# A two-part schedule of a recurrence and dense layers: new order tables, a ring of decay rates with 10 places in place of 11, half as many products of r and v

## The reference

```python
def _attn_ref(r, k, v, w, a, b):            # 4 batches, 8 heads, 768 steps, 40 wide
    state = zeros((B, H, D, D))
    for t in range(S):
        y[:, :, t] = einsum('bhd,bhde->bhe', rt, state)
        Sa = einsum('bhde,bhe->bhd', state, at)
        state_decay = state * wt[:, :, None, :] - einsum('bhd,bhe->bhde', Sa, bt)
        state = state_decay + einsum('bhd,bhe->bhde', vt, kt)
def _moe_ref(x, w_in, w_out):               # 3072 x 320 -> 2048 -> 320
    h = x @ w_in
    g = where(h >= 1, h, where(h <= -1, 0, (h + 1) ** 2 / 4))
    return g @ w_out
def _moe2_ref(x, w1, w2, w3, w_out):        # 3072 x 320 -> 768 -> 320
    return maximum(maximum(x @ w1, x @ w2), x @ w3) @ w_out
```

## Time and profile before

| | us |
|---|---|
| median of 3 runs | 1052.78 |
| lowest, highest | 1052.1, 1056.64 |
| the profiled execution | 1052.78 |
| its span, first to last instruction | 1051.1 |
| TensorE busy | 962.9 (92%) |
| VectorE, ScalarE, GpSimd busy | 506.8, 393.1, 456.5 |
| mean granted TensorE clock | 0.97 of 2.4 GHz |

### The profile page before, as it was taken

How to read it: one execution, slowest core, us unless ns; L and a number is a source line. 1 busy time by engine, 2 the same in 40 slices (tenths; PEclk the granted TensorE clock), 3 DMA queues, 4 the chain that set the end, 5 groups by cost and what they waited for, 6 DMA issues and landing times.

```text
span 1051.1 us, 29793 instructions
## 1 busy us (share of the span) xinstructions
PE 962.9 (92%) x12330; PEld 807.1 (77%) x12330; DVE 506.8 (48%) x700; ACT 393.1 (37%) x719; POOL 456.5 (43%) x633
## 2 busy tenths in 40 slices
PE   6648999899998887899999999999999999999998
PEld 5436787788776776677888788878887888888887
DVE  8886666667552452696333323332333243324321
ACT  1214455455554563464233323332333133313321
POOL 3586786959688841242133213321332133123311
PEclk9957999999998899999999999999999999999999
DMA  5854667676645631462000100010001000100000
GB/s 84 142 108 89 119 104 133 102 139 107 128 81 116 116 72 28 135 181 68 1 26 1 31 1 26 0 30 0 25 0 30 0 25 0 30 0 26 0 1 26
DMA packets 242915, 61.27 MB, mean 58 GB/s; under 512 B 223728, under 2 KB 238832, under 8 KB 242800
## 3 DMA queue, kind: packets, MB, share of 16 engines
q1 hardware_dynamic: 147760, 44.86, 19.3%
q10 hardware_dynamic: 95040, 14.76, 8.6%
HBM read 44.89 MB, written 14.68 MB: 57 GB/s over the span
## 4 chain that ended last, share of the span: by engine, by line
issue 27%; PE 17%; POOL 10%; DVE 3%; ACT 1%; DMA 1%; POOLq 0%; DVEq 0%; ACTq 0%; SPq 0%
POOL hid_lo L1399 10%; PE ring L1212 8%; PE acc L1212 5%; PE ring L1222 3%; PE ring L1254 2%; DVE sq L1457 1%; PE acc L1276 1%; DVE clip L1451 1%; DMA raw<-in_moe_w_dram 1%; DVE wmax_lo L1425 1%; ACT sq L1361 0%; ACT hid_hi L1337 0%; POOLq L35 0%; DVE win_lo L1425 0%; DVE wout_lo L1417 0%
## 5 line engine op out<-in xcount | busy, mean ns | idle before, releaser
L1399 POOL TENSOR_TENSOR hid_lo<-sq,hid_hi 128x512 fp32r<-128x512 f32 x132 | 174.4, 1321 | 453.5 <-ACT hid_hi L1337 453.5
L1451 DVE TENSOR_SCALAR clip<-ring 128x512 f32<-128x512 f32 x96 | 66.2, 690 | 132.1 <-PE ring L1222 132.1
L448 POOL TENSOR_TENSOR prod<-sysX 128x30 f32<-128x30 f32 (+14 forms) x193 | 101.8, 527 | 58.1 <-DMA sysX<-systems 42.8
L1337 ACT CAST hid_hi<-sq 128x512 fp32r<-128x512 f32 x132 | 82.0, 622 | 93.5 <-DVE sq L1457 71.5
L1361 ACT ACTIVATE sq<-clip 128x512 f32<-128x512 f32 x96 | 60.7, 633 | 147.7 <-DVE clip L1451 145.9
L452 POOL TENSOR_TENSOR sysX<-sysX,prod 128x30 f32<-128x30 f32 (+14 forms) x193 | 106.9, 554 | 15.1
L1457 DVE SCALAR_TENSOR_TENSOR sq<-clip,sq 128x512 f32<-128x512 f32 x96 | 67.9, 708 | 59.9 <-ACT sq L1361 59.9
L1212 PE MATMUL acc<-hid_hi,wout_hi 128*128 128x512 f32 x192 | 76.4, 398 | 7.7 <-POOL hid_lo L1399 7.6
L1482 DVE TENSOR_TENSOR sq<-ring,clip 128x512 f32<-128x512 f32 x36 | 24.9, 692 | 120.4 <-PE ring L1222 98.1
L1383 ACT COPY clip<-ring 128x512 f32<-128x512 f32 x36 | 21.1, 587 | 153.8 <-PE ring L1222 153.8
L1212 PE MATMUL ring<-x_hi,win_hi 128*128 128x512 f32 x192 | 75.5, 393 | 3.4 <-PEq L958 3.4
(11 more groups left out here) (166 smaller groups left out, 2177.4 us busy)
## 6 DMA issues: line engine op xcount, KB each, us to landing
nat_k<-in_k_dram ACTq DMA_DIRECT2D x48, 80.0 KB, 3.4
vz<-in_v_dram SPq DMA_DIRECT2D x96, 40.0 KB
nat_r<-in_r_dram SPq DMA_DIRECT2D x96, 40.0 KB, 2.8
xT<-yT SPq DMA_DIRECT2D x96, 40.0 KB
out_dram<-res SPq DMA_DIRECT2D x24, 160.0 KB, 1.8
inverses_T<-sysX SPq DMA_DIRECT2D x7, 512.0 KB, 4.5
nat_w<-in_w_dram ACTq DMA_DIRECT2D x44, 80.0 KB
nat_a<-in_a_dram ACTq DMA_DIRECT2D x44, 80.0 KB, 3.5
```

The lines of the kernel that those rows point to most:

```text
L448: g_.tensor_tensor(some, X[:, 0:j, j:j + 1].to_broadcast([P, j, rest]), X[:, j:j + 1, j + 1:BLK].to_broadcast([P, j, rest]), ALU.mult)\
L1337: nc.scalar.copy(hid[(u if u < T1 else u - T1) % HB][0][:, :], src).then_inc(hid_hi, 1)
L1399: nc.gpsimd.tensor_tensor(hid[at % HB][1][:, :], sq[at % 2][:, :], f32(hid[at % HB][0][:, :]), ALU.subtract)\
L1451: nc.vector.tensor_scalar(clip[f % 2][:, :], ring[(f + 2) % 4][:, :], -1.0, None, ALU.max).then_inc(clipped, 1)
```

## The change: what it does

- ORDER, FINISH, START, SOLVE_FROM, SOLVE_AT, FIRST_STEP and BANK get other contents. Stages w, a, b, n run 9, 8, 8, 8 pieces ahead in place of 10, 9, 9, 9; dn stays at 9 on TensorE and goes from 9 to 8 on VectorE. On GpSimd a round has 12 steps in place of 9, and a unit's solving starts later.
- The ring `rates` has EARLY (10) places in place of 11; every wait that named RATED names EARLY.
- rr does one product with a weight tile of 64 rows and 128 columns where it did two with 64 by 64: 32 products a piece in place of 64.
- VectorE's steps of unit 1 write to a tile of their own, `prod_v`, in place of `xsum`, and the wait of x(0) for these steps is gone. They start one short round earlier.

```diff
-EARLY, RATED, LATE = 10, 11, 3
+EARLY, LATE = 10, 3
-        rates = ring("rates", RATED, [P, RATES + DM])
+        rates = ring("rates", EARLY, [P, RATES + DM])
-        prod = sb("prod", [P, (BLK // 2) ** 2])
+        prod, prod_v = (sb(n, [P, (BLK // 2) ** 2]) for n in ("prod", "prod_v"))
         ORDER = {
-            "PE": [("g", 0), ("p", 0), ("gs", 0), ("qt", 0), ("dn", 9), ("z", 0), ("ys", 0), ("w", 10), ("yt", 0),
-                   ("vz", 0), ("k", 1), ("a", 9), ("r", 2), ("rr", 0), ("b", 9), ("ak", 1), ("st", -1), ("n", 9),
-                   ("xy", 0)],
-            "ACT": [("load w1", 10), ("load b0", 10), ("load b1", 9), ("load k0", 2), ("rates", 0), ("load k1", 2),
-                    ("p", 0), ("gs", 0), ("qt", 0), ("inverse", 0), ("z", 0), ("w", 10), ("vz", 0), ("r", 2),
-                    ("load w0", 11), ("k", 1), ("load a0", 10), ("b", 9), ("load a1", 11), ("st", -1), ("dense", -1)],
-            "DVE": [("ak", 0), ("inverse", 0), ("x", -1), ("scan", 9), ("y", -1), ("bk", 0), ("dn", 9), ("a", 9),
-                    ("bn", 9), ("dense", -1), ("rr", 0), ("n", 9)],
-            "POOL": [("step", 0), ("step", 0), ("step", 0), ("step", 0), ("step", 0), ("stTc", -1), ("step", 0),
-                     ("step", 0), ("total", -1), ("step", 0), ("step", 0), ("kn", 2)],
-            "SP": [("load v0", 1), ("load r1", 2), ("solved", 1), ("system", 8), ("load r0", 2), ("unit", 8),
-                   ("y", -1), ("inverse", 1), ("load v1", 2), ("dense", -1)],
+            "PE": [("g", 0), ("w", 9), ("a", 8), ("p", 0), ("gs", 0), ("qt", 0), ("b", 8), ("z", 0), ("n", 8),
+                   ("dn", 9), ("vz", 0), ("k", 1), ("r", 2), ("ys", 0), ("rr", 0), ("yt", 0), ("ak", 1), ("st", -1),
                    ("xy", 0)],
+            "ACT": [("inverse", -1), ("w", 9), ("p", 0), ("gs", 0), ("load k1", 3), ("qt", 0), ("b", 8), ("z", 0),
+                    ("load w1", 10), ("vz", 0), ("load a0", 9), ("load k0", 3), ("load b1", 10), ("k", 1), ("r", 2),
+                    ("rates", 0), ("st", -1), ("load a1", 10), ("load b0", 10), ("dense", -1), ("load w0", 11)],
+            "DVE": [("dn", 8), ("rr", -1), ("ak", 0), ("bn", 8), ("inverse", 0), ("x", -1), ("y", -1), ("a", 8),
+                    ("scan", 9), ("n", 8), ("bk", 0), ("dense", -1)],
             "POOL": [("step", 0), ("step", 0), ("step", 0), ("step", 0), ("step", 0), ("stTc", -1), ("step", 0),
+                     ("total", -1), ("step", 0), ("kn", 2), ("step", 0), ("step", 0), ("step", 0), ("step", 0),
+                     ("step", 0)],
+            "SP": [("load r0", 2), ("solved", 1), ("load v1", 1), ("y", -1), ("inverse", 1), ("system", 8),
+                   ("load v0", 2), ("unit", 8), ("dense", -1), ("load r1", 3)],
...
         START = {
-            "PE": [("n", 7), ("a", 5), ("w", 4), ("r", 15), ("dn", 5), ("k", 19), ("ak", 19), ("b", 6)],
+            "PE": [("dn", 4), ("ak", 19), ("a", 3), ("w", 2), ("b", 4), ("k", 18), ("n", 4), ("r", 15)],
-            "DVE": [("step", 0), ("a", 1), ("scan", 0), ("step", 0), ("dn", 1), ("n", 2), ("bn", 1)],
+            "DVE": [("step", 0), ("a", 1), ("step", 0), ("n", 2), ("dn", 1), ("bn", 1), ("scan", 0)],
...
-        VECTOR_STEPS, VECTOR_FROM = 17, 10
+        VECTOR_STEPS, VECTOR_FROM = 17, 9
-        SOLVE_FROM, SOLVE_AT = [3, 3, 5, 4, 4, 4, 8], 0
+        SOLVE_FROM, SOLVE_AT = [3, 3, 4, 4, 4, 4, 5], 7
...
                 for used in (out["y"], stT_made, rates_checked, out["a"]):
-                    ge(dve, used, g - RATED + 1)
-                ge(dve, done["dn"], g - RATED + 1)
+                    ge(dve, used, g - EARLY + 1)
+                ge(dve, done["dn"], g - EARLY + 1)
...
-                        for to in range(2):
-                            for i in range(2):
-                                at = (j * HP + m) * CH
-                                last = nc.tensor.matmul(ps[rows(to), i, at:at + CH], vzT[rows(i), j, m, rows(to)],
-                                                        rT[g % LATE][rows(i), m, j, :], start=True, stop=True)
+                        for i in range(2):
+                            at = (j * HP + m) * CH
+                            last = nc.tensor.matmul(ps[:, i, at:at + CH], vzT[rows(i), j, m, :],
+                                                    rT[g % LATE][rows(i), m, j, :], start=True, stop=True)
...
-                if g == 0:
-                    dve.wait_ge(sys_step[1], 2 * VECTOR_STEPS)
...
-                some = xsum[:, :, :, :].rearrange("r j p d -> r (j p d)")[:, 0:j * rest]\
-                    .rearrange("r (m t) -> r m t", m=j)
+                some = prod_v[:, 0:j * rest].rearrange("r (m t) -> r m t", m=j)
```

More of the change, by code:

```diff
@@ L133, in attention @@
+            "POOL": [("step", 0), ("kn", 1), ("step", 0), ("step", 0), ("total", 0), ("step", 0), ("step", 0),
+                     ("step", 0), ("stTc", 11), ("step", 0), ("step", 0), ("step", 0), ("step", 0), ("step", 0)],
+            "SP": [("unit", 11), ("solved", 5), ("system", 7), ("load r1", 8), ("load v1", 4), ("inverse", 12),
+                   ("load r0", 13), ("load v0", 11), ("dense", 12), ("y", 11)],
         }
         START = {
[4 rows of a table removed]
-            "POOL": [("kn", 9), ("step", 0), ("step", 0), ("step", 0), ("step", 0)],
@@ L140, in attention @@
-            "SP": [("system", 3), ("load v1", 5), ("unit", 3), ("load r0", 7)],
[4 rows of a table added]
+            "POOL": [("step", 0), ("step", 0), ("kn", 14), ("step", 0)],
+            "SP": [("unit", 1), ("load r1", 5), ("inverse", 53), ("solved", 152), ("load v1", 34), ("load r0", 0),
+                   ("system", 0), ("load v0", 10)],
         }
         START_LEN, FINISH_FROM = 20, 21
-        VECTOR_STEPS, VECTOR_FROM = 17, 10
-        FIRST_STEP = {0: 0, 1: 203}
-        SOLVE_FROM, SOLVE_AT = [3, 3, 5, 4, 4, 4, 8], 0
+        VECTOR_STEPS, VECTOR_FROM = 17, 9
@@ L146, in attention @@
+        FIRST_STEP = {0: 0, 1: 349}
+        SOLVE_FROM, SOLVE_AT = [3, 3, 4, 4, 4, 4, 5], 7
         OPENS = {"gs": "g", "xy": "ys"}
@@ L148, in attention @@
         READERS = {"xy": ("x", "y")}
-        BANK = {"g": 1, "p": 4, "qt": 4, "dn": 0, "z": 1, "ys": 2, "w": 4, "vz": 1, "k": 0, "a": 3, "r": 4, "rr": 1,
-                "b": 4, "ak": 0, "st": 3, "n": 1}
+        BANK = {"g": 1, "w": 4, "a": 0, "p": 3, "qt": 4, "b": 3, "z": 0, "n": 1, "dn": 3, "vz": 0, "k": 1, "r": 4,
+                "ys": 2, "rr": 0, "ak": 1, "st": 4}
         bank_of = {n: (pair + single)[at] for n, at in BANK.items()}
@@ L221, in attention @@
                 last[BANK[n]] = next((c for c, o in OPENS.items() if o == n), n), g
-        raw = [rates[g % RATED][:, 0:PIECE] for g in (14, 15, 16)]
+        raw = [rates[i][:, 0:PIECE] for i in (4, 5, 6)]
         def decay(g):
-            return rates[g % RATED][:, 0:RATES].rearrange("r (p j t) -> r p j t", p=HP, j=2)
+            return rates[g % EARLY][:, 0:RATES].rearrange("r (p j t) -> r p j t", p=HP, j=2)
         def recip(g):
-            return rates[g % RATED][:, RATES:]
+            return rates[g % EARLY][:, RATES:]
         def rows(half, n=CH):
@@ L529, in dn @@
                     at = (2 * p + 1) * (CH + 1) - CH + 1
-                    nc.tensor.transpose(ps[:, 0, p * P:(p + 1) * P], rates[g % RATED][:, at:at + P], ident[:, :])
+                    nc.tensor.transpose(ps[:, 0, p * P:(p + 1) * P], rates[g % EARLY][:, at:at + P], ident[:, :])
                     last = nc.tensor.transpose(ps[rows(0), 0, p * P:(p + 1) * P], decay(g)[:, p, 0, 1:CH + 1],
@@ L759, in check_rates @@
                 act.wait_ge(out["dn"], g + 1)
-                squares(rates[g % RATED][:, :], 0, g, rates_checked)
+                squares(rates[g % EARLY][:, :], 0, g, rates_checked)
             def check_inverse(g):
@@ L812, in scan @@
                 for used in (out["y"], stT_made, rates_checked, out["a"]):
-                    ge(dve, used, g - RATED + 1)
-                ge(dve, done["dn"], g - RATED + 1)
-                nc.vector.tensor_tensor_scan(rates[g % RATED][:, 0:RATES],
+                    ge(dve, used, g - EARLY + 1)
+                ge(dve, done["dn"], g - EARLY + 1)
+                nc.vector.tensor_tensor_scan(rates[g % EARLY][:, 0:RATES],
                                              wT[:, :, :, :].rearrange("r p j t -> r (p j t)"),
```

## The result

| | us |
|---|---|
| before, median of 4 runs on the same chip | 1052.44 (1049.81 to 1056.64) |
| after, median of 4 runs | 1086.57 (1085.18 to 1091.22) |
| ratio | 1.0328, 95% interval 1.0283 to 1.0375 |
| the profiled execution of after, its span | 1080.92, 1079.2 |

The change makes the kernel 3.3% slower. The forecast was 1062, slower by 0.9%: the sign is right, the size is not, and 1087 lies outside the range.

A forecast was written before the change was run, and what follows sets the result against it. TensorE, plus its in-order waits, was taken to bound rounds 0 to 14. 1052.8 - 6.2 (tables) + 0 (rr) + 8.1 (ring) + 2.4 (clock) + 1.8 (START) + 2.9 (end) = 1061.8, say 1062; range 1047 to 1070.

The forecast's parts named there:

- tables: Rounds 0 to 14: named TensorE waits go, leaving 0.46 of 1.32 us a round; 14.64 becomes 14.2, -6.2 us.
- START: Opening short rounds, about 6 us each; VectorE reaches its steps at 58 to 60, rr(0) 1.8 us later.
- the end: Rounds 15 onward and FINISH: an extra a, and ys and yt covering less, +2.9 us.
- shorter ring: Rounds 4, 8, 12: GpSimd's decayed state starts 5.7 us late, scan and dn wait, 2.7 us each, +8.1.
- slower clock: TensorE behind the three stalls: work runs at a slower granted clock, 0 to 5.4 us, taken as +2.4.
- rr: TensorE's rr in 24 pieces: half as many products at double the time each (31 ns), +1.4 at most, taken as zero.
- Rival C: rr is bound by the number of products: -11 us, 1041 without and 1051 with the stalls; chance 0.06.
- Rival A: GpSimd's lag stays within the cover, so no stalls: 1051, no change; chance 0.27.
- price list: TensorE's stage times summed per round without waits: 13.32 us before, 13.74 after, so 0.42 longer.
- Rival B: No late decayed state on GpSimd and the new round loses its waits altogether: 1045; chance 0.11.
- Rival D: START is the worse loss, each 1 us a short round more costing 8 us; with the stalls 1070; chance 0.10.

The follow-up runs named there:

- experiment 4: The kernel before with the new tables alone (64 products, 11 places, VectorE's first steps in `xsum`): 1061.02 us, 1.0073.
- 2: The changed kernel with only rr set back to 64 products: 1070.03 us, 1.0127.
- experiment 3: The changed kernel with the ring of rates back at 11 places and VectorE's first steps in `xsum` again: 1074.09 us, 1.0179.
- experiment 1: The kernel before with only rr changed to 32 products of a 64x128 weight: 1058.61 us, 1.0073.
- Experiment 8: The changed kernel with nine solving steps a round on GpSimd in place of 12, the last three taken out: 1102.69 us, 1.0473.
- 11: The kernel before with ScalarE's rates check moved from ahead of load k1 and p to behind w: 1053.34 us, 1.0006.
- 12: The kernel before with ScalarE's rates check behind load a0, ahead of b, and load k1 behind p: 1052.97 us, 0.9986.
- 9: The kernel before with the new tables alone, ys and yt put back between z and vz on TensorE: 1058.76 us, 1.0059.
- 10: The changed kernel with ys and yt put back between z and vz on TensorE: 1074.73 us, 1.0207.
- 5: The kernel before, rr's 64 products reordered, all of the upper row half before the lower: 1058.43 us, one execution.
- experiment 6: The kernel before, rr with 32 products of 64x128, all of one row half before the other: 1118.3 us, one execution.

## Why the forecast was wrong

By its own steps, with the size that the runs of single parts give:

| step | forecast | measured | from |
|---|---|---|---|
| tables, START and the end | -6.2 + 1.8 + 2.9 = -1.5 | +8.4 | experiment 4 |
| shorter ring, with its slower clock | +8.1 + 2.4 = +10.5 | +9.0, +12.5 | 4 to 2; 3 to after |
| rr | 0 | +6.0; +16.5, +13.1 | before to 1; 2 to after, 4 to 3 |

**rr: the step that failed most.** I took k's row, 0.40 for 8 products, and subtracted a fixed start of 0.15 from it before dividing. That gave 31 ns a product. The start came from groups whose products lie in four or sixteen parts of the array; nothing in the earlier trace rows showed that the wide form has one. Without it the same row gives 0.40/8 = 50 ns, with the shown length 0.47/8 = 59, and 60 was measured. The bounds were too tight for the same reason: I had called 31 ns the worst. The 0.84 a piece (2.00 in place of 1.16) is 20.2 us of TensorE time in 24 pieces, and by the medians the change costs 6.0 us in the old tables and 13.1 to 16.5 in the new. Of the 20.2, 11.8 fall in rounds 0 to 14, and there the stage table shows almost nothing: +2.2 (before), +0.2 (tables, long ring) and +2.2 (after). The longer rr filled waits: TensorE's idle time in these rounds falls from 14.0 us to 7.6, from 19.2 to 9.3 and from 24.2 to 15.1. In the kernel before those for r and `inv` go, in the new tables those for k's copy (5.2 us in experiment 4, none among the waits of experiment 3 and 0.2 in after). In rounds 20 to 23 it shows in full and more: 3.6 to 6.2 us for 2.5 of products. Rival C, that the number of products binds, falls (half as many take longer). The Trainium skill's 60 cycles a product (TensorEngine Tiling (Array Packing), Performance Considerations) would have made rr 0.8 us shorter a piece, an estimate from that page; it is 0.84 longer.

What stays open: by the profiled executions rr costs 7.9 us in after (1079.2 - 1071.3) and not 16.5. These two executions lie at opposite ends of their kernels' times, so part is scatter; which stage the remaining microseconds fall in no trace here shows.

**The ring: the mechanism right, the slower clock too small.** The lag was put at 5.7 us and measured at 5.7, the stall at 2.7 and measured at 2.9 at most (8.3 in three), in three rounds. The slower clock behind them was undersized: the three rounds are 56.4 us, and three of the others would be 43.5, so 12.9 less 8.3 leaves 4.6, against 2.4; the stretches behind the gaps, at a granted clock of 0.64, show 1.4 each of it. The rounds are the forecast's, 4, 8 and 12. Rival A (lag within the cover) falls. Experiment 8 adds what I had not seen: with nine steps in place of 12 and the same start a unit is late, since GpSimd's 55 us of work fill four rounds of 57.

**The tables: wrong sign.** The -6.2 stood on the removal of named waits, and was too large even by them: 5.0, 1.8 and 1.8 us are 0.61 a round, which leaves 0.71 of the 1.32 and not 0.46: rounds of 14.45, and so -2.7. In after they were removed: `low` falls from 5.0 to 0.4, and those for r and `inv` are gone. But with 64 products (experiment 4) only `low` goes, `inv` stays at 1.5 us and r grows to 4.3; k's copy and z come on top, and the same 14 rounds take 204.5. My price list named only what stood ahead of p on ScalarE and SyncE; the three load issues that were moved between vz and k were not counted, though ScalarE is idle for 20.1 us behind them, ahead of k. Experiments 11 and 12 point the same way in the kernel before: 2.0 and 4.2 us less wait at the place of `low` are worth nothing that a median shows. Rival B (no late stT, no waits) falls with them.

**The end: undersized.** I gave ys and yt behind vz 0.2 a round; the earlier trace rows show 0.19 idle with them in front, and I read that as the price. It was what was left after their cover; without it the wait is 1.0 a round. With the clock at 0.87 the stretch costs 9.1 us in the profiled execution of experiment 4 and 7.5 in after's. With ys early it is 79 us in both (experiments 9 and 10); by the medians that is worth 11.8 us in after, and 2.3, within the scatter, in the tables alone. The forecast had 2.9 for all that comes behind round 14.

**START: the time near, the way to it not.** rr(0) at 94.8, forecast 95.4. But the eight rounds of START are 6.8 us apart (first reciprocal 11.54, last 59.33), not 6, and VectorE reaches its steps at 63.4, not 58 to 60 (60.2 in the kernel before). VectorE's timeline of after has dn(8) ahead of ak and the small transpose, 1.4 to 2 us later than in the earlier trace rows, as forecast:

```profile
80.96 2.15 DVE L824 RECIPROCAL rates<-single 128x320 f32<-128x320 f32 x1
83.02 0.63 DVE L851 TENSOR_TENSOR ak<-pair,pos 128x512 f32<-128x512 f32 x1
...
84.26 0.43 DVE L809 STREAM_TRANSPOSE inv<-invT 128x256 f32<-128x256 f32 x1
```

rr(0) moves by up to 4.6 us between kernels whose START tables are the same, so that the sum agrees is partly luck. Rival D (1070 from a worse START) gave a time that is nearer, by a cause that did not occur.

No kernel here beats the kernel before by more than the scatter.

## What to carry to other kernels

Price a product from a row with the same weights, the same streamed columns and the same parts of the array side by side, and don't subtract from such a row a start that was fitted to groups of another form. A wait that a table removes is worth nothing until the trace shows what the engine would wait for next in the same round; take one edit away at a time, on both sides, before adding terms. Where an engine's work fills its rounds, its burst needs slack in a ring: 11 places gave it here, 10 did not.

## What was not expected of the hardware

- Four 64 x 64 products in the four quarters of the array take 68 ns together, a single 64 x 128 product 104; alternating the halves of the rows brings the wide one to 60 (experiments 1, 5, 6).
- A longer TensorE stage can be almost free while it falls into waits: 11.8 us more of products in 14 rounds cost 0.2 to 2.2 in the profiled executions. It stopped being free when they grew further: experiment 6 has 19.5 us more than experiment 1 there (14 times 1.39) and its rounds 0 to 14 take 236.0 against 207.2, 28.9 more.
- The granted clock of rounds 14 to 20 goes with the gaps more than with the work in these kernels: 0.91 before, 1.00 with the longer rr (experiment 1), 0.87 in after, 0.98 with ys early. These are the windows of before and of experiment 1, which has more TensorE work and takes less time there:

```profile
298.50:378.80 80.30, 68.34 (x2102) 57.82 (x2100) 32.60 (x50) 42.87 (x90) 70.19 (x123) 0.91 0.52 99
```

```profile
298.90:376.30 77.40, 68.38 (x1910) 58.79 (x1908) 32.98 (x50) 42.75 (x89) 69.11 (x123) 1.00 0.54 101
```

Gaps aren't all of it. Experiment 6, with all of one half of the rows before the other, is granted 0.92 in rounds 0 to 14 with TensorE busy 98.6% of the time; no run shows why.

```profile
94.70:330.70 236.00, 232.74 (x5089) 202.76 (x5088) 134.45 (x169) 107.23 (x222) 146.30 (x251) 0.92 0.56 102
```
